# The last layer's output for two token tiles by seven products of quarters, and two small tables of powers by loads

## The reference, cut to what matters

```python
# linear attention with decay, blocks of 64 tokens, 2 x 8 heads of 64, 768 tokens each
intra = einsum(qb, kb) * Dmask          # Dmask[i, j] = lam ** (i - j), lower triangle
inter = (qb * lam_pow) @ kv_state       # lam_pow[i]  = lam ** (i + 1)
kv_state = lam ** 64 * kv_state + (kb * rev_pow).T @ vb   # rev_pow[i] = lam ** (63 - i)
x = attn_out as [1536, 512]
g = leaky(x @ w_in);  y = g @ w_out     # hidden width 2048, leaky = max(0.01 h, h)
a = y @ w1;  b = y @ w2                 # hidden width 1024
out = ((a * b) @ w3) @ w_out2           # width 1024, then 512
```

## Time and profile before

| | us |
|---|---|
| median of 3 runs (lowest, highest) | 518.74 (518.65, 519.13) |
| the profiled execution | 517.97 |
| its span | 516.2 |
| PE busy | 511.6 (99%) |
| DVE busy | 323.8 (63%) |
| ACT busy | 193.4 (37%) |
| POOL busy | 93.6 (18%) |

### The profile page before, as it was taken

How to read it: one execution, slowest core, us unless ns; L and a number is a source line. 1 busy time by engine, 2 the same in 40 slices (tenths; PEclk the granted TensorE clock), 3 DMA queues, 4 the chain that set the end, 5 groups by cost and what they waited for, 6 DMA issues and landing times.

```text
span 516.2 us, 9088 instructions
## 1 busy us (share of the span) xinstructions
PE 511.6 (99%) x3604; PEld 422.6 (82%) x3604; DVE 323.8 (63%) x494; ACT 193.4 (37%) x342; POOL 93.6 (18%) x101
## 2 busy tenths in 40 slices
PE   8999999999999999999999999999999999999997
PEld 7788888888888888888888888888888888888886
DVE  5767356767777876686755887697777753322332
ACT  5454243443456533333312456333333215232221
POOL 2223132112212321122200031222233200000000
PEclk9999999999999999999999999999999999999999
DMA  8998582434121111111100113221122111101502
GB/s 285 352 395 262 198 296 90 151 123 126 41 89 36 43 39 42 41 42 41 43 0 1 52 50 75 69 62 61 63 61 62 41 43 41 42 29 54 203 2 81
DMA packets 25370, 49.37 MB, mean 96 GB/s; under 512 B 3680, under 2 KB 3688, under 8 KB 25328
## 3 DMA queue, kind: packets, MB, share of 16 engines
q1 hardware_dynamic: 22848, 41.17, 24.4%
q10 hardware_dynamic: 2448, 7.62, 4.5%
q0 software_dynamic: 32, 0.00, 0.0%
HBM read 43.53 MB, written 5.25 MB: 95 GB/s over the span
## 4 chain that ended last, share of the span: by engine, by line
PE 99%; ACT 0%; DVE 0%; issue 0%; DVEq 0%
PE acc L1255 14%; PE acc L1256 13%; PE acc L1257 13%; PE hid L1467 10%; PE hid L1468 10%; PE hid L1466 10%; PE hid L1255 7%; PE hid L1256 7%; PE hid L1257 7%; PE hid L1287 1%; PE hid L1302 1%; PE hid L1315 1%; PE hid L1326 1%; PE hid L1352 1%; PE acc L1571 1%; PE acc L1569 1%
## 5 line engine op out<-in xcount | busy, mean ns | idle before, releaser
L1255 PE MATMUL acc<-g_hi,wb 128*128 128x512 f32 x276 | 107.8, 391 | 0.0
L1257 PE MATMUL acc<-g_hi,wb 128*128 128x512 f32 x276 | 107.4, 389 | 0.0
L1256 PE MATMUL acc<-g_lo,wb 128*128 128x512 f32 x276 | 107.4, 389 | 0.0
L1255 PEld LDWEIGHTS acc<-g_hi,wb 128*128 128x128 f32 x276 | 51.8, 188 | 11.0
L1257 PEld LDWEIGHTS acc<-g_hi,wb 128*128 128x128 f32 x276 | 51.8, 188 | 10.7
L1256 PEld LDWEIGHTS acc<-g_lo,wb 128*128 128x128 f32 x276 | 51.8, 188 | 10.6
L623 POOL TENSOR_TENSOR w_in_lo_place<-stage 128x256 f32<-128x256 f32 x16 | 12.8, 797 | 211.4 <-PE hid L1468 121.0
L1255 PE MATMUL hid<-xy_hi,wa_hi 128*128 128x512 f32 x128 | 50.2, 393 | 0.0
L1257 PE MATMUL hid<-xy_hi,wa_lo 128*128 128x512 f32 x128 | 49.8, 389 | 0.0
L1256 PE MATMUL hid<-xy_lo,wa_hi 128*128 128x512 f32 x128 | 49.8, 389 | 0.0
L1466 PE MATMUL hid<-wa_hi 128*128 128x512 f32 x128 | 49.8, 389 | 0.0
(11 more groups left out here) (176 smaller groups left out, 813.7 us busy)
## 6 DMA issues: line engine op xcount, KB each, us to landing
stage<-weights SPq DMA_DIRECT2D x109, 256.0 KB, 3.0
w_out_place<-attn ACTq DMA_DIRECT2D x12, 512.0 KB, 4.8
outT<-x_hi_place SPq DMA_DIRECT2D x11, 256.0 KB, 3.0
x_hi_place<-attn SPq DMA_DIRECT2D x4, 512.0 KB, 8.6
w_out_place<-attn SPq DMA_DIRECT2D x4, 512.0 KB, 7.5
w_dram<-x_lo_place SPq DMA_DIRECT2D x8, 256.0 KB, 5.4
stage<-w_dram SPq DMA_DIRECT2D x8, 256.0 KB, 2.7
x_lo_place<-attn SPq DMA_DIRECT2D x2, 512.0 KB, 6.8
```

The source lines that it names most:

```text
L1255: nc.tensor.matmul(out, w_hi, a_hi, start=first, stop=False)
L1256: nc.tensor.matmul(out, w_hi, a_lo, start=False, stop=False)
L1257: return nc.tensor.matmul(out, w_lo, a_hi, start=False, stop=final)
```

## The change

There are two parts.

**A. The output for token tiles 1 and 2.** The output of these two tiles is [512 output columns] x [1024 tokens], a sum over 8 rows f of 128. It is cut in quarters: two halves of the output columns (d = 0, 1 and d = 2, 3), two halves of the rows (f = 0 to 3 and 4 to 7), and the two token tiles. Seven products of quarters stand in place of eight. Each is 4 rows x 2 output tiles x 3 matmuls = 24 matmuls. Two of them (`first_step_of_out`) use plain weights and g1(f), and stand between the gates of token tile 2; five (`out_product`) follow after them. They need four sums of quarters of w34 (S1 to S4, `make_sum34`), for which SP loads all of w34 again (`raw34`, eight times 256 KB), and four differences and sums of gated tiles for each of 4 rows (T1 to T4, `make_right`). All of these are made and split to lo by DVE and rounded by ACT, inside the loop over the gates. The sums of weights are handled as 128 x 1024. The partial outputs are joined by DVE (`second_made` to `last_made`), and the very last tile is added and stored in two halves. `out_step(1, f)` is gone from before the gates.

**B. The tables of powers.** The small matmuls, `head_selector` and DVE's two copies are gone. SP loads `q_pow` from `pow_dram` with two more DMAs behind those of `decay`; the keys' factors are read from `decay` itself. `SEGMENTS` changes, so that the first stretch holds 20 products and the second 8.

```diff
-SEGMENTS = [16, 10, 12, 10, 10, 6]
+SEGMENTS = [20, 8, 10, 10, 10, 6]
-SPLIT_AGAIN = (1, 3)
-LAST_TOGETHER = 3
+ROWS = F2 // 2
+MAKE_SUMS34 = (1, 2)
+ROUND_SUMS34 = {2: 2, 3: 2}
+SPLIT_SUMS34 = {3: 2, 6: 2}
+FIRST_OUT = ROWS
...
 SP
+            for hh in range(2):
+                of_head = bass.AP(pow_dram, 2 * BLOCK * hh + BLOCK, [[0, D], [4 * BLOCK, PAIRS], [1, BLOCK]])
+                sp.dma_start(q_pow[half(hh), :, 0, :], of_head).then_inc(q_pow_loaded, 16)
...
+                if ORDER[w] == ("again", 3):
+                    wait_then_step(g1_ready, F2)
+                    for f in range(F2):
+                        sp.dma_start(raw34(f), w34_dram.ap()[f]).then_inc(raw34_loaded, 16)
...
 ACT, in the loop over f = 1 to 7 (again_set: the two tiles of set f + 2)
+                round_gated(N1 + F2 + f, g1_ready, f + 1, g1(f))
                 copy_gate(f)
                 if f + 2 < F2:
+                    w = again_set()
+                for i in range(ROUND_SUMS34.get(f, 0)):
+                    sums34_hi(2 * (f - 2) + i)
+                if f == FIRST_OUT:
+                    for d in range(2):
+                        copy_first(d)
+                for t in [T1] if f < ROWS else [T2, T3, T4, B22]:
+                    right_hi(t, f % ROWS)
...
 DVE
+            for f in range(1, F2):
                 split_gated(N1 + F2 + f, g1(f))
                 gate(f)
                 if f + 2 < F2:
+                    w = again_set()
+                if f in MAKE_SUMS34:
+                    for i in [(S1, S3), (S2, S4)][f - 1]:
+                        make_sum34(i)
+                for t in [T1] if f < ROWS else [T3, T2, T4]:
+                    make_right(t, f % ROWS)
+                for t in [T1] if f < ROWS else [T2, T3, T4, B22]:
+                    right_lo(t, f % ROWS)
+                for _ in range(SPLIT_SUMS34.get(f, 0)):
+                    sums34_lo(j)
+                    j += 1
...
+            dve.wait_ge(pair_ready, 8 + 2)
+            for cols in (slice(0, WIDE), slice(WIDE, TOK)):
+                nc.vector.tensor_tensor(second_of_out(1)[:, cols], z_bank[1][:, cols], second_of_out(1)[:, cols],
+                                        ALU.add).then_inc(last_made, 1)
...
 PE
-            pe.wait_ge(selector_loaded, 16)
-            pe.wait_ge(pow_chain, POW_STEPS)
-            for p in range(PAIRS):
-                nc.tensor.matmul(q_spread[:, p, :], selector[:, p, :], pow_row[:, BLOCK:2 * BLOCK], start=True, stop=True)
...
-            for f in range(F2):
-                out_step(1, f)
...
+            for f in range(1, F2):
+                if f > 1:
+                    pe.wait_ge(gate_ready, f - 1)
+                gate(f, 0)
+                gate(f, 1).then_inc(hid_ready, 1)
+                first_step_of_out(f - 1)
+            first_step_of_out(F2 - 1)
...
+            pe.wait_ge(s34_split, ROWS)
+            pe.wait_ge(gate_ready, F2 - 1)
+            for d in range(2):
+                out_product(z_bank[d], S1, T1, d, True)
+            pe.wait_ge(out_ready, KD_TILES)
+            for d in range(2):
+                out_product(y_bank[:, d, :], S2, T2, d, True)
+            for d in range(2):
+                pe.wait_ge(second_made, d + 1)
+                out_product(y_bank[:, d, :], S3, T3, d, False)
...
```

More of the change, by code:

```diff
@@ L318, in g1, with gated @@
             return w_out_place[:, 7, f - STAGE + STAGE_LEFT, :]
[L321 to L327, removed]
+        def gated(f):
+            if f < ROWS:
+                return x_lo_place[:, f, tokens(0)]
+            return wb_place(AGAIN_OUT + f - ROWS, 1)
@@ L889, in _, with again_set @@
                 round_gated(N1 + f, g0_ready, f + 1, g[:, f % 2, :])
+            def again_set():
+                for i in range(2):
+                    weight_hi(w + i)
+                return w + 2
+            w = again_set()
             copy_gate(0)
@@ L937, in weight_lo @@
                 lo_part(lo, staged_tile(w, lo), hi, split_done)
[L939 to L944, removed]
+            for w in range(len(EARLY_34)):
                 weight_lo(w)
@@ new lines, in right_lo @@
+            def right_lo(t, row):
+                dve.wait_ge(right_hi_done, SPLIT_G[t, row] + 1)
+                if t != T1:
+                    dve.wait_ge(right_made, MADE_G[T4, row] + 1)
+                hi, lo = parts_of_g(t, row)
+                lo_part(lo, exact_of_g(t, row), hi, right_split)
+            w = again_set()
+            gate(0)
+            split_gated(N1 + F2, g1(0))
+            w = again_set()
+            make_right(T1, 0)
+            right_lo(T1, 0)
+            j = 0
@@ L1365, in _ @@
                                  stop=False).then_inc(w34_done, 1)
-            pe.wait_ge(selector_loaded, 16)
-            pe.wait_ge(pow_chain, POW_STEPS)
-            for p in range(PAIRS):
-                nc.tensor.matmul(q_spread[:, p, :], selector[:, p, :], pow_row[:, BLOCK:2 * BLOCK], start=True, stop=True)
-            for b in range(2):
-                last = nc.tensor.matmul(k_spread[half(b), :], pow_row[:, BLOCK - 1:2 * BLOCK - 1], selector[:, :, 0:P:D],
-                                        start=True, stop=True, skip_group_check=True)
-            last.then_inc(pow_spread, 1)
             w34_products(HALF, first_product(1))
@@ L1548, in _ @@
             out_step(0, F2 - 1)
-            for f in range(F2):
-                out_step(1, f)
             pe.wait_ge(g0_ready, F2)
             pe.wait_ge(z_used, 2 * STEPS)
-            for f in range(F2):
-                if f + 1 < F2:
-                    if f > 0:
-                        pe.wait_ge(gate_ready, f)
-                    gate(f + 1, 0)
-                    gate(f + 1, 1).then_inc(hid_ready, 1)
-                if f < F2 - LAST_TOGETHER:
-                    out_step(NT - 1, f)
@@ new lines, in _, with left34 @@
+            for f in range(1, F2):
[5 more added lines that the diff above has]
+            first_step_of_out(F2 - 1)
+            def left34(i, row, d):
+                if i == A22:
+                    cols = slice(WIDE + d * P, WIDE + (d + 1) * P)
+                    return [wb[:, w34_slot(ROWS + row), part, cols] for part in range(2)]
+                cols = slice(WIDE * ((i - S1) % 2) + d * P, WIDE * ((i - S1) % 2) + (d + 1) * P)
+                return [wa[:, 2 * row + (i - S1) // 2].rearrange("p k m -> p (k m)")[:, cols] for wa in (wa_hi, wa_lo)]
@@ new lines, in out_product @@
+            def out_product(out, left, t, d, first):
+                for row in range(ROWS):
+                    pe.wait_ge(right_split, SPLIT_G[t, row] + 1)
+                    w_hi, w_lo = left34(left, row, d)
+                    a_hi, a_lo = parts_of_g(t, row)
+                    nc.tensor.matmul(out, w_hi, a_hi, start=first and row == 0, stop=False, skip_group_check=True)
+                    nc.tensor.matmul(out, w_lo, a_hi, start=False, stop=False, skip_group_check=True)
+                    last = nc.tensor.matmul(out, w_hi, a_lo, start=False, stop=row == ROWS - 1, skip_group_check=True)
+                last.then_inc(pair_ready, 1)
@@ L1587, in source_of @@
+            for d in range(2):
+                pe.wait_ge(third_made, 2 * d + 2)
+                out_product(z_bank[d], S4, B22, d, False)
 def source_of(name):
```

275 lines of the change are left out of this document (186 added, 89 removed).

## The result

The changed kernel takes 520.73 us (median of 5 runs, 518.40 to 521.52), the kernel before beside it 518.74 (5 runs, 518.65 to 519.13): a ratio of 1.0033, 95% interval [1.0021, 1.0046]. It is slower by 0.33%, and 5.6 us above the forecast of 515.1. Its profiled execution is the fastest of the five, 518.40 (span 516.5); 514.4 was forecast for it.

What follows compares the result with a forecast made beforehand. PE, busy 99% of the span, was taken as the bound. Part A's matmuls -5.44, new wait +2.55, part B -0.82 and the end +0.1 gave -3.6: 518.74 to 515.1 us, 8-in-10 range 512.4 to 517.4.

Steps and rivals of the forecast that it cites:

- gain of part A: Output of token tiles 1 and 2 on PE: 24 fewer matmuls at 0.2267 us, -5.44 us.
- DVE's count: From row 1's gate to the split of g1(7): DVE needs 43.7 us, so PE waits 2.55 us.
- lower end: Low case of PE's new wait: DVE distances of 0.60 and 1.05 us give 1.6 us.
- wait of row 2: In DVE's chain: DVE waits while ACT has two casts of 1024 ahead in row 2, 1.95 us.
- Rival 2: DVE's operations stand a full row apart, 0.69 and 1.23 us: 3.7 us more, 518.8 us; 8%.
- The hold costs nothing with 3 us left.: SP's loads of w34 delay weight tiles 4 and 5, but they come 3 us before PE's need: no cost.
- rival 3: PE's pause lowers its clock: 2.1 us lost at half speed, 517.2 us; 8%.
- forecast's own wait: PE waits for DVE's split of g1(7) in front of the last first_step_of_out: 2.55 us.
- Part B, -0.82: At the start, the second group of products begins at 8.45 instead of 9.27: -0.82 us.
- tiles 12 and 13: Weight tiles pushed by two added issues: cast by ACT at 19.2, split by 21.1, wanted at 23.3.
- The end, +0.1: After the last matmul: two half-size DVE adds cost +0.15, a half-size DMA saves at most 0.3; taken as +0.1 us.
- Rival 5: DVE's chain so late, 47.3 us or more, that the clock falls too: slower, 520.9 us; 5%.

Runs made afterwards that it cites:

- experiment 6: Changed kernel with rounding and splits of T3, T4 and B22 moved behind row 7: 513.94 us; part A only, so edited and with w34 loads later: 513.19 us.
- experiment 7: Both parts, those splits deferred, w34 loads later: 513.83 us; ACT's w34 copies also moved ahead: 512.98; part A only with all three edits: 514.33.
- experiment 3: Changed kernel with 16 extra matmuls, whose result nothing reads, placed in PE's wait: 518.47 us, ratio 0.9995.
- experiment 5: Kernel before with chained DVE operations added ahead of a split PE waits for: six 522.20 us (ratio 1.0074), eight 523.86 us (1.0107).
- experiment 1: Each part of the change by itself against the kernel before: part B 519.30 us (ratio 1.0016), part A 519.63 us (1.0018).
- experiment 2: Kernel before with part B only, and ACT's copy of w34 moved ahead of a weight tile's cast: 517.72 us, ratio 0.9979.
- A alone: Changed kernel with part B undone, so the start of the kernel before: 519.63 us, ratio 1.0018 to the kernel before.
- B alone: Kernel before with only part B added (tables of powers by loads, segments 20 and 8): 519.30 us, ratio 1.0016.
- experiment 4: Changed kernel with the eight loads of w34 issued after weight tiles 4 and 5 instead of ahead of them: 518.63 us, ratio 1.0006.
- part A with all repairs: Part A with the start as before, T3, T4 and B22 splits deferred, w34 loads later, ACT's w34 copies ahead: 514.33 us, ratio 0.9924.

## Why the prediction was wrong

- **The gain of part A, 24 x 0.2267 = 5.44.** Right: experiment 6 has it in full.
- **DVE's count.** Right (only its lower end was not: with distances of 0.60 and 1.05 the count gives a wait of 1.3 us, not 1.6): 43.7 us forecast, 44.0 measured; the distance of large operations and the wait of row 2 (1.95 forecast, 1.99 measured) too. Rival 2, full rows apart, is refuted, and with it the rule of the Trainium skill, "VectorE: DVE Perf Modes", section "The DRAIN you can't avoid", taken at its word; its own exception, that an operation not held starts earlier, is what the 1.13 us of 1.22 show.
- **"The hold costs nothing with 3 us left."** Failed, +0.7 of the 1.05 us by which the pause is longer (2.9 us with the loads later, 3.6 with them early). The 3 us were counted up to PE's need of tiles 4 and 5. But the next need was DVE's, which had to finish all it could ahead of its chain, because from 437 us on DVE was the bound. The other 0.3 us is the chain's 44.0 instead of 43.7. With DVE's order mended, no cost of the hold can be told (experiment 7).
- **The pause and the clock.** The step that failed was to let the wait cost its length, and to give rival 3 only 8% since "the pause is short". It was no rival but a companion of the forecast's own wait: +1.7 in the profiled execution, 2.0 by experiment 3, 1.5 to 2 on top of 2.3 and of 3.8 us by experiment 5. Rival 3's own price, 2.1 us, came close partly by luck: it takes all of 1.47 to 5.65 us as slow, but the eight rows up to 4.90 have another shape, the granted clock in these windows reads 1.00, and the twelve full-size matmuls from 4.90 to 8.03 lose only 3.13 - 12 x 0.2267 = 0.4 us. The rule of the Trainium skill, "TensorE: Matmul & The Clock Gate", section "Part 1: The HAM clock gate", that an idle engine falls to half clock and must earn it back, agrees with the windows above; that it can do so after as little as 2.3 us is what they add.
- **Part B, -0.82.** The gain at 8.3 us is real (0.82), and attention's start was unharmed (19.39 against 19.6). What failed is the step that priced the pushed loads: it looked at tiles 12 and 13 for PE and found slack, and did not look for what else stands behind the cast of a later tile on ACT. +0.8 instead (experiment 1), and -1.0 with the order mended (experiment 2). In the profiled execution of the change that wait did not appear. PE's lead over the kernel before fell by 0.35 us between 26 and 36 us, and by 0.7 in the pause near 96 us for which no releaser shows and which every kernel with part B has. The forecast had no term for that pause, and its cause stays open.
- **The end, +0.1.** The last matmul starts 512.73, the span ends 3.8 us later, against 3.4 before: +0.35.

For the profiled execution: wait +1.05, clock +1.7, start +0.9, end +0.25, around the span +0.1, together 4.0, which is 518.4 - 514.4. The median lies 2.3 us above that execution (0.8 before). Its runs show 0.993 where the profiled one shows 0.997; a stretch of 3.5 us at half speed is 1.75 / 516 = 0.0034 of the mean clock, so they had about two such stretches. Where the second one lies was not seen, since only the profiled execution has rows. That it follows the wait near 31 us is likely and not shown: A alone never has less than 0.996, B alone has one run at 0.997, which is 2.5 us above its median, and 0.993 or 0.990 occur only where both halves are in. Rival 5 gave 520.9 and the kernel takes 520.73, but that is luck: it comes through more and smaller terms than a late chain. Its condition was also off by its own count: with the clock's 2.1 us in it, wait plus clock pass 6.2 us when the chain is 45.2 us long, not 47.3. It was 44.0.

## What to carry to other kernels

Before work is moved from the bound engine to another, put that engine's whole program in the order in which the bound engine needs the results; here the same instructions in a better order turn +0.33% into -0.8%, and with two more moves into -1.1%. A pause of TensorE of 2 to 4 us is to be priced at its length plus up to 2 us: in all runs of experiment 5 and of A alone the clock fell, but with a pause of 2.2 us in B alone the clock stayed at 1.00 or 0.999 in 11 of 12 runs, and with one of 2.9 us in 3 of 12 (only the profiled run of each has rows; that the pause is alike in the others is assumed). One profile does not show which it will be. Slack of a load is counted at the first engine in its path that has no time to spare, and for every instruction that stands behind its user in an in-order program, also those that need no load.

## What the runs showed of the hardware

- The granted clock can fall after a pause of 2.3 us, and only 1.5 us after PE resumed (445.09 to 446.62); with a pause of 3.6 us in the changed kernel it was low at once, and with one of 4.3 us in A alone 0.6 us after. Pauses of 2.2 us (B alone, profiled) and of 2.9 us (experiment 4, profiled) left it at 1.00. After a fall matmuls are 0.427 apart instead of 0.227 for about 3.4 us.
- The same opening takes up to 1.2 us more or less from execution to execution (its last pair starts 7.22 to 8.38), while the 416 us behind it repeat within 0.1 us where the program is the same (415.96 to 416.03 in five kernels that start like the kernel before).
- PE's pauses marked "issue", of 0.2 to 1.0 us among small matmuls or ahead of a large one, come and go with code that is otherwise the same at that place: none in the kernel before and with part A alone, 0.2 to 0.5 in the kernels that have part B, 1.0 in part A with all repairs. They cost more than the list says: the 0.4 near 96 us cost 0.7. No run settled their cause.
